# Attention, two mixtures of experts: raw weights by GpSimd, and the attention stage in another order

## What is computed

```python
# attention: 24 chunks of 32 queries; each sees 8 memory keys and up to 16 + 32 + 8 keys around it
scores = scale * np.matmul(q_c, k_full.transpose(0, 1, 3, 2))
scores = scores - np.max(scores, axis=-1, keepdims=True)
a = np.exp(scores)
a = a / (np.sum(a, axis=-1, keepdims=True) + 1e-09)
out[:, :, c_start:c_end] = np.matmul(a, v_full)
...
# dense layer; x_prev is x shifted by one row
xk = mu_k * x + (1.0 - mu_k) * x_prev
xr = mu_r * x + (1.0 - mu_r) * x_prev
k = np.maximum(xk @ w_k, 0.0)
v = k * k @ w_v
r = 1.0 / (1.0 + np.exp(-(xr @ w_r)))
return (r * v).astype(np.float32)
...
# experts: e is the row's own best expert or the one carried from the row before
h = np.maximum(x[b, s] @ w1[e], 0.0)
out[b, s] = p[e] * (h @ w2[e])
```

## Time and profile before

| | |
|---|---|
| median of 3 runs | 530.2 us (527.29 to 530.47) |
| profiled execution | 529.36 us |
| its span | 527.6 us |
| granted TensorE clock, mean | 0.913 |
| TensorE matmuls busy | 441.3 us (84%) |
| VectorE, ScalarE, GpSimd busy | 246.1, 212.0, 55.5 us |
| attention stage | up to 81.30 us |
| mix stage | from 81.30 us to about 240 us |

### The profile page before, as it was taken

The page is one execution under the profiler, slowest core; times in us unless marked ns, Lnnn a source line. Parts: engine busy times, 40 slices in busy tenths (PEclk is TensorE's granted clock), DMA queues, the critical chain, the costliest instruction groups (busy, mean ns, idle before and its releaser), DMA issues.

```text
span 527.6 us, 10195 instructions
## 1 busy us (share of the span) xinstructions
PE 441.3 (84%) x3759; PEld 367.4 (70%) x3759; DVE 246.1 (47%) x477; ACT 212.0 (40%) x319; POOL 55.5 (11%) x62
## 2 busy tenths in 40 slices
PE   1767649999999999999930079999999999999993
PEld 1545538899898989889820057777777777777772
DVE  2566783433544343253056149222472247465961
ACT  1345482624434353443012047222452255555750
POOL 0000000020101001010004601111111111111110
PEclk9876677999999999999965569999999999999997
DMA  8789930063000000000006689511173128383810
GB/s 317 268 277 343 322 118 1 1 260 140 0 0 0 0 0 0 0 1 1 1 0 198 201 296 414 207 40 40 60 238 121 40 79 251 138 267 121 267 64 10
DMA packets 18457, 67.31 MB, mean 128 GB/s; under 512 B 2750, under 2 KB 2878, under 8 KB 18432
## 3 DMA queue, kind: packets, MB, share of 16 engines
q1 hardware_dynamic: 13248, 50.92, 27.8%
q0 software_dynamic: 4896, 16.05, 8.8%
q10 hardware_dynamic: 288, 0.02, 0.0%
HBM read 55.41 MB, written 12.62 MB: 129 GB/s over the span
## 4 chain that ended last, share of the span: by engine, by line
PE 73%; DMA 11%; issue 6%; DVE 4%; POOL 3%; ACT 0%; SPq 0%; POOLq 0%; DVEq 0%; ACTq 0%
PE PS L537 16%; PE PS L409 13%; PE PS L520 13%; PE PS L441 12%; PE PS L425 6%; DMA VV<-tiles 5%; DMA XR<-grouped_rows 4%; POOL grouped_rows L1102 3%; PE PS L528 2%; PE PS L459 2%; PE PS L511 2%; PE PS L336 1%; PE PS L374 1%; DMA QK<-tiles 1%; PE PS L349 1%
## 5 line engine op out<-in xcount | busy, mean ns | idle before, releaser
L1017 DVE TENSOR_TENSOR ELO<-ERAW,EHI 128x1024 fp32r<-128x1024 f32 x56 | 66.8, 1220 | 12.5 <-ACT EHI L698 9.9
L698 ACT ACTIVATE EHI<-ERAW 128x1024 fp32r<-128x1024 f32 x56 | 57.7, 1054 | 29.6 <-DMA ERAW<-wexp 20.7
L409 PE MATMUL PS<-XHI,WHI 128*128 128x256 f32 x192 | 56.3, 293 | 0.8 <-issue 0.8
L537 PE MATMUL PS<-EHI,HH 128*128 128x512 f32 x128 | 54.6, 426 | 2.6 <-issue 1.0
L409 PE MATMUL PS<-XLO,WHI 128*128 128x256 f32 x192 | 54.9, 286 | 0.0
L409 PE MATMUL PS<-XHI,WLO 128*128 128x256 f32 x192 | 54.9, 286 | 0.0
L520 PE MATMUL PS<-EHI,XSH 128*128 128x512 f32 x128 | 53.0, 414 | 1.4 <-DVE XSL L1025 1.4
L1038 DVE TENSOR_TENSOR HL<-PS,HH 128x512 fp32r<-128x512 f32 x32 | 22.1, 691 | 66.3 <-ACT HH L718 65.9
L520 PE MATMUL PS<-ELO,XSH 128*128 128x512 f32 x128 | 51.5, 402 | 0.0
L520 PE MATMUL PS<-EHI,XSL 128*128 128x512 f32 x128 | 51.4, 401 | 0.0
L537 PE MATMUL PS<-EHI,HL 128*128 128x512 f32 x128 | 50.6, 395 | 0.0
(11 more groups left out here) (141 smaller groups left out, 778.7 us busy)
## 6 DMA issues: line engine op xcount, KB each, us to landing
ERAW<-wexp SPq DMA_DIRECT2D x56, 512.0 KB, 6.4
QK<-tiles SPq DMA_DIRECT2D x12, 768.0 KB, 6.3
VV<-tiles SPq DMA_DIRECT2D x12, 520.0 KB, 6.1
grouped_rows<-ZR POOLq DMA_DIRECT2D x1, 5140.0 KB, 17.3
RAW<-wmix SPq DMA_DIRECT2D x10, 512.0 KB, 5.3
XR<-grouped_rows POOLq DMA_DIRECT2D x17, 257.0 KB, 4.3
CO<-consts SPq DMA_DIRECT2D x1, 406.0 KB, 4.9
rows_out<-OSB,OIDX POOLq DMA_INDIRECT x16, 4.0
```

The source lines that it names most:

```text
L409: last = nc.tensor.matmul(PS[q % 2][:, half * 256:half * 256 + 256], w[:, c:c + P], x[:, k, :], start=n == 0, stop=n == 11)
L537: last = nc.tensor.matmul(PS[4][:, :], x[:, f, :], ww[:, c:c + D], start=n == 0, stop=n == 23)
L698: nc.scalar.activation(EHI[w][:, c * CH2:(c + 1) * CH2], ERAW[c][:], ACT.Copy).then_inc(ehi_done, 1)
L1017: nc.vector.tensor_tensor(ELO[w][:, c * CH2:(c + 1) * CH2], ERAW[c][:], EHI[w][:, c * CH2:(c + 1) * CH2].bitcast(F32), ALU.subtract).then_ ...
```

## The change

- The RAW loads go from SP's queue to GpSimd's, written out with fixed addresses. Block 0 waits for the scores of tile 1, block 1 for those of tile 2, block n for WLO of block n-2.
- SP's order becomes V of t+2, then QK of t+4.
- TensorE's waits for V and for QK stand at the values and at the scores that read them, no longer ahead of the transposed probabilities. An increment of a new semaphore, for which nothing waits, follows each.
- TensorE's order for tile t becomes transposed probabilities of t, transposed x of t-1, values of t, scores of t+2.
- VectorE's order becomes `normed(t)`, `shifted(t+2)`, `weight_lo(t-2)`.
- The streams of ScalarE and VectorE for this stage are written out for all 12 tiles instead of looped. The mix of pair 0 goes to tiles 6 and 7 (`mix_scaled`, `mix_full`) and 8 and 9 (`mix_hi`, `mix_lo`), at the end of each tile's calls.
- `wlo_done` no longer starts at 2; the waits for it change by 2.

```diff
 SP
             def ahead(t, u):
+                sp.wait_ge(pv_done, t + 1)
+                v_load(t + 2, u)
                 sp.wait_ge(scores_done, t + 3)
                 qk_load(t + 4, u)
-                sp.wait_ge(pv_done, t + 1)
-                v_load(t + 2, u)
-                raw_next(t, u)
 TensorE
             def scores(t, u, first):
...
                     pe.wait_ge(sub_done, t - 1)
+                    pe.wait_ge(qk_loaded[u], 8 * (t - u) + 16)
+                    pe.sem_inc(passed_pe, 1)
...
-            def probs_transposed(t, u, first, more):
+            def probs_transposed(t, u, first):
                 pe.wait_ge(exp_done, t + 1)
-                pe.wait_ge(v_loaded[u], 8 * (t - u) + 16)
-                if more:
-                    pe.wait_ge(qk_loaded[u], 8 * (t + 2 - u) + 16)
...
             def values(t, u, first):
                 pe.wait_ge(pt_evac, t + 1)
+                pe.wait_ge(v_loaded[u], 8 * (t - u) + 16)
                 if not first:
                     pe.wait_ge(norm_done, t)
+                pe.sem_inc(passed_pe, 1)
...
-                    probs_transposed(t, u, first and u == 0, not last)
-                    if not last:
-                        scores(t + 2, u, False)
+                    probs_transposed(t, u, first and u == 0)
                     if not (first and u == 0):
                         x_transposed(t - 1, 1 - u, first and u == 1)
                     values(t, u, first and u == 0)
+                    if not last:
+                        scores(t + 2, u, False)
 ScalarE
+            def attention(t):
+                u = t % 2
+                probs_out(t, u, t < 2)
+                if t:
+                    x_out(t - 1)
+                if t + 2 < NT:
+                    exps(t + 2, u, False)
+                if t >= 2:
+                    weight_hi(t - 2)
+                if t in (6, 7):
+                    mix_scaled(0, t - 6, True)
+                if t in (8, 9):
+                    mix_hi(0, t - 8, True)
 VectorE
+            def attention(t):
+                u = t % 2
+                normed(t, u, t < 2)
+                if t + 2 < NT:
+                    shifted(t + 2, u, False)
+                if t >= 2:
+                    weight_lo(t - 2)
+                if t in (6, 7):
+                    mix_full(0, t - 6, True)
+                if t in (8, 9):
+                    mix_lo(0, t - 8, True)
 GpSimd
+            for n in range(N1):
+                if n >= 2:
+                    pool.wait_ge(wlo_done, n - 1)
+                else:
+                    pool.wait_ge(scores_done, n + 2)
+                pool.dma_start(RAW[n % 2][:], wmix[:, n * CH1:(n + 1) * CH1]).then_inc(raw_loaded[n % 2], 16)
             pool.wait_ge(x2_done, 1)
```

More of the change, by code:

```diff
@@ L159, in moe_program @@
         tables_in = sem("tables_in")
+        passed_pe = sem("passed_pe")
         qk_loaded = [sem(f"qk_loaded{i}") for i in range(2)]
@@ L253, in v_load @@
                              ).then_inc(v_loaded[u], 16)
-            def raw_load(n, u):
-                sp.dma_start(RAW[u][:], wmix[:, ds(n * CH1, CH1)]).then_inc(raw_loaded[u], 16)
             qk_load(0, 0)
@@ L262, in _ @@
             v_load(1, 1)
-            def raw_next(n, u):
-                sp.wait_ge(wlo_done, n + 1)
-                raw_load(n, u)
             def ahead(t, u):
+                sp.wait_ge(pv_done, t + 1)
+                v_load(t + 2, u)
                 sp.wait_ge(scores_done, t + 3)
                 qk_load(t + 4, u)
-                sp.wait_ge(pv_done, t + 1)
-                v_load(t + 2, u)
-                raw_next(t, u)
             for t in range(2):
@@ L285, in _ @@
                 v_load(NT - 2 + u, u)
-                raw_next(N1 - 2 + u, u)
             sp.dma_start(CO[:, C_LT:CW], consts[:, C_LT:CW]).then_inc(tables_in, 16)
@@ L391, in _ @@
             x_transposed(NT - 1, 1, False)
-            pe.wait_ge(wlo_done, N1A + 2)
+            pe.wait_ge(wlo_done, N1A)
             pe.wait_ge(xt_evac, NT)
@@ L416, in gate @@
                 if first:
-                    pe.wait_ge(wlo_done, N1A + KT * D // CH1 + 2)
+                    pe.wait_ge(wlo_done, N1A + KT * D // CH1)
                 else:
@@ L437, in down @@
                     if first and c % CH1 == 0:
-                        pe.wait_ge(wlo_done, c // CH1 + 3)
+                        pe.wait_ge(wlo_done, c // CH1 + 1)
                     r = slice(u * P, u * P + P)
@@ L591, in x_out, with weight_hi @@
                                      ACT.Copy).then_inc(xt_evac, 1)
[L593 to L596, removed]
+            def weight_hi(n):
+                act.wait_ge(raw_loaded[n % 2], 16 * (n // 2 + 1))
+                nc.scalar.activation(WHI[:, n * CH1:(n + 1) * CH1], RAW[n % 2][:],
                                      ACT.Copy).then_inc(whi_done, 1)
[L599 to L613, removed]
+            def attention(t):
[11 more added lines that the diff above has]
+                    mix_hi(0, t - 8, True)
             def mix_scaled(g, kind, first):
@@ L640, in _ @@
             exps(1, 1, True)
-            over_pairs(act, attention)
+            for t in range(NT):
+                attention(t)
             x_out(NT - 1)
@@ L802, in normed, with weight_lo @@
                 last.then_inc(norm_done, 1)
-            def weight_lo(n, u):
-                dve.wait_ge(const_in, 48)
+            def weight_lo(n):
                 dve.wait_ge(whi_done, n + 1)
-                nc.vector.tensor_tensor(WLO[:, ds(n * CH1, CH1)], RAW[u][:], WHI[:, ds(n * CH1, CH1)].bitcast(F32),
+                c = slice(n * CH1, (n + 1) * CH1)
+                nc.vector.tensor_tensor(WLO[:, c], RAW[n % 2][:], WHI[:, c].bitcast(F32),
                                         ALU.subtract).then_inc(wlo_done, 1)
@@ L847, in _ @@
             dve.wait_ge(setup_done, 1)
-            dve.sem_inc(wlo_done, 2)
             shifted(0, 0, True)
             shifted(1, 1, True)
-            over_pairs(dve, attention)
+            for t in range(NT):
+                attention(t)
             dve.sem_inc(logit_evac, 1)
```

## The result

The changed kernel takes 534.09 us in the median of five runs (533.84 to 536.82), against 530.2 us before (five runs by now, 526.76 to 530.47): 1.0105 times, with a 95% interval of 1.0068 to 1.0142. It is slower by 3.9 us by the medians and by 5.6 us by the ratio, whose interval reaches from 3.6 to 7.5 us; forecast were 537 us and a range from 531 to 542. The profiled execution took 533.84 us, 4.5 us more than before, with a span of 531.6 us, 4.0 us more; the other 0.5 us lies outside the span (2.2 us instead of 1.8). It does so in every kernel whose RAW loads GpSimd issues, 2.1 to 2.3 us, while the three with these loads on SP's queue have 1.8. The mix stage's first matmul (L401, before L409) comes at 84.28 us instead of 81.30, so 3.0 of the 4.0 us are the attention stage's. The last 1.0 us lies behind it, in stages that the change leaves alone.

The account below looks back on a forecast made before the run. Loads and TensorE shared the bound before; a chain of 6.15 us a tile would replace 5.48. Start, eight tiles, mix 5.2, gap 2.5 and end put the mix stage's first matmul at 88.4 us, forecasting 537 us, range 531 to 542.

Parts of the forecast that it names:

- The ring: Attention stage: a closed chain from values(t) through VectorE and ScalarE to values(t+1) sets the tile time, 6.15 us.
- Loads out of the bound: Attention stage: TensorE and the DMA engines go idle, DMA share near 0.8 instead of 0.93.
- The mix is moved, not hidden: Tiles 6 to 9: pair 0's mix falls between WHI and the next PTS on ScalarE, still costing 5.2 us.
- The sum: Attention stage's terms added up to the mix stage's first matmul: 88.4 us, 7.1 us later than 81.30.
- the gap: TensorE's unexplained stop, before in tile 5's scores, expected to stay, in tile 3's values: 2.5 us, between 0 and 2.5.
- tile 10 to tile 11: From the values of tile 10 to those of tile 11: bounds 2.9 and 3.8 us, taken 3.4.
- the rest: From the values of tile 11 to the mix stage's first matmul: 4.44 us, as before.
- my slack for it: Start, scores of tile 2: RAW(0) beside their QK load delays it, taken 0.7 us, bound 1.5 us.
- rival 2: Attention stage: tile chain at its low end of 5.85 us, stop gone, 530.6 us, no change; 28% with all within 1%.
- The skill's sum: Whole kernel, with TensorE's 2.5 us stop not due in straight code, as fetching is mostly hidden: 534.5 us.
- Rival 1: Attention stage: the chain doesn't bind, freed loads win, 5.04 us a tile, 9.6 us earlier, 520.6 us; 8%.
- Rival 3: Attention stage: RAW comes late from GpSimd's queue, beyond 9.8 us; at 12 us it costs 9 us, 546; 5%.

Follow-up runs that it names:

- both cures: Changed kernel with TensorE's, VectorE's and SP's orders of before, and ScalarE's weight_hi and mix ahead of exps: 521.79 us, 0.9896 times before.
- waits alone: Kernel before, with only the waits for V and QK moved to the values and scores that read them: 524.5 us, 0.9944 times before.
- orders of before: Changed kernel with TensorE's scores of t+2 ahead of values of t and VectorE's shifted ahead of normed again: 526.15 us, 0.9958 times before.

## Why the prediction was right

- **The ring.** Predicted 5.99 to 6.31 us, taken 6.15; measured 6.07 in the mean of the four plain ones. That it is the cause is shown from both sides: it comes with the two orders alone, and it goes when the work in it goes.
- **Loads out of the bound.** DMA share forecast near 0.8, measured 0.71 to 0.79; and with 4 MB less of loads the tiles stay where they were.
- **The mix is moved, not hidden.** Predicted 5.2 us in the rings; measured 29.76-4x6.07=5.5 us, and 8.46-3.55=4.9 us as a lump at the end.
- **The sum.** Predicted 88.4, measured 84.28 us for the first matmul of the mix stage, 4.1 us too much. The terms: values of tile 1 at 17.84 instead of 18.5, -0.7; tile 2 5.18 behind, 0; the eight rings and the mix 77.07-23.02=54.05 instead of 54.4, -0.35; the gap, 0 instead of 2.5; tile 10 to tile 11 3.55 instead of 3.4, +0.15; the rest 3.66 instead of 4.44, -0.8, since the last values and transposes were shorter, as at the higher clock (0.86 and 0.66 us instead of 1.18 and 1.11). The 0.7 us are RAW(0) and my slack for it: the scores of tile 2 started at 13.62, right behind the values, and its QK load took 6.2 us to land in both profiles. So the turns between queues, which the Trainium skill ("DMA: Bandwidth & Descriptors", Queues, rings and completion order) describes, cost this load nothing that the profile shows; the next QK load, on its way with RAW(0), took 7.16 us instead of 6.46, and nothing waited for it.
- **Luck in the total.** The first matmul came 4.1 us earlier than forecast, the profiled time only 2.7 us (533.84 against 536.5): 1.0 us behind that matmul and 0.5 outside the span, for both of which I had put nothing, offset part of the miss. The median was 0.25 us above the profiled run and not 0.8. The lower interval bound is a ratio of 1.0068, within the 1% that I had called no change, and half of rival 2 came true: the gap was gone, though the ring was not at its low end of 5.85.
- **The term that was wrong** is the gap of 2.5 us. "Nothing that I see removes it" overlooked that the ring itself might. The gap shows in three profiles, before (31.80), with both cures and with the waits alone, each time in the scores of tile 5, with three to five of the recorded matmuls left. A second one of its kind stands 126 recorded matmuls ahead of it each time, in the values of tile 2. In the kernel with the waits at their own matmuls:

```profile
22.43 0.24 PE L365 MATMUL PS<-VV,PTS 64*32 64x65 f32 x1
25.80 1.06 PE L365 MATMUL PS<-VV,PTS 64*32 64x65 f32 x63 [3.12 <-issue]
...
31.72 0.31 PE L339 MATMUL PS<-QK 64*32 64x64 f32 x5 [2.77 <-issue]
```

With both cures:

```profile
28.67 0.43 PE L329 MATMUL PS<-QK 64*32 64x64 f32 x5 [1.85 <-issue]
```

A fixed count of instructions points at their supply, and the profile records that too: a DMA queue of the kind "instruction" moves 16 KB in one packet, five times between 10 and 38 us in each profile. Here it is in the kernel before, from 29.40 to 30.52 us (packets, MB, share):

```profile
q8 instruction: 1, 0.02, 6.0%
```

The table sets each stop beside the packet that ends during it or shortly before:

| kernel, where TensorE stops | idle, us | packet, us | TensorE goes on | after the packet's end |
|---|---|---|---|---|
| before, values of tile 2 | 0.22 | 23.37 to 24.43 | 25.79 | 1.36 |
| before, scores of tile 5 | 2.54 | 29.45 to 30.53 | 31.80 | 1.27 |
| waits alone, values of tile 2 | 3.12 | 23.42 to 24.42 | 25.80 | 1.38 |
| waits alone, scores of tile 5 | 2.77 | 29.32 to 30.36 | 31.72 | 1.36 |
| both cures, values of tile 2 | 1.35 | 21.41 to 22.39 | 23.67 | 1.28 |
| both cures, scores of tile 5 | 1.85 | 26.22 to 27.27 | 28.67 | 1.40 |

The two places lie some 470 and 596 matmuls from the start of the stream (two fewer where the waits add instructions), in every kernel. In none of the 13 profiles does TensorE pass one of them less than 1.2 us after the end of the packet that belongs to it. In the changed kernel the second packet ends at 26.18, and some 1.3 us more make 27.5. TensorE stands idle from 26.6 to 29.14 ahead of the values of tile 3, waiting for PTS, and passes the place within these values at 29.77, so it never notices. In the open kernels without a gap (RAW by GpSimd, orders of before) it passes the second place 1.49 and 1.34 us after the packet's end, just late enough. So the gap is TensorE waiting for instructions, as far as times can show it, and a kernel in which TensorE waits for something else shortly before doesn't pay it. No run moved such a packet by itself.

The Trainium skill ("Runtime: NRT & Kernel Launch", Instruction fetch mechanics) calls this fetch mostly hidden; in ten of the profiles it is, in three it costs 1.85 to 2.77 us at the second place, which lies in the first pass of TensorE's loop, ahead of any jump back. I had kept the gap on the strength of its row. The skill's sum, 534.5, came nearer to 534.09, but by the same luck as above: without the gap the first matmul was still forecast 1.6 us too late, and 1.5 us were missing behind it.

- **Rival 1** (the freed loads win) didn't come true, for the reason given, the order in ScalarE's code; its time, 520.6, is about what the kernel takes in which WHI no longer stands between PR and PTS (521.73). **Rival 3** fell: RAW took 4.8 us in the median, and WHI waited for it once, 0.43 us.

## What to carry to other kernels

Before moving a step behind another, follow the orders of all engines once round from a step to the same step of the next tile, and add up the links: if every link waits for the one before, the sum is the tile time, whatever the busy shares say. Then look for work in the ring that isn't of the ring (here WHI and the mix) and put it where that engine waits; here this turned a change that cost 1% into one that gains 1.2%. Two edits can each close the same ring, so undo them together, or neither shows.

## What the runs showed of the hardware

**RAW loads from GpSimd's queue are no faster than from SP's.** With only the queue changed, in the kernel before, the 512 KB take 6.6 us to land in the median, against 5.3. The 4.8 us of the changed kernel come with a lower DMA share (0.71 to 0.79 instead of 0.93); the kernel with the new orders and RAW on SP's queue has 4.2 us.

**TensorE can run out of instructions.** A stream of small matmuls stood still for up to 3.12 us until 1.27 to 1.40 us after a 16 KB packet of the instruction queue had ended.
